# Scores of the next head pair ahead of VectorE's maxima, and w_out first in the queue, in a fused attention and two-MoE kernel

## What is computed

```python
q_d, k_d, v_d = (mean over groups of 4 positions of q, k, v)
out_up = np.repeat(sm_attn(q_d, k_d, v_d), 4, axis=2)      # pooled attention
mask = np.abs(pos[:, None] - pos[None, :]) < 4             # local attention
x = out_up + softmax(where(mask, q @ k.T / 8, -1e9)) @ v   # -> [2304, 512]
h = (sigmoid(x @ w_gate) * (x @ w_val)) @ w_out            # [2304, 512]
logits = h @ phi                                           # [2304, 32]
slots = softmax(logits, axis=0).T @ h                      # [32, 512]
slot_out[e] = relu(slots[e] @ w1[e]) @ w2[e]               # 8 experts, 4 slots each
out = softmax(logits, axis=1) @ slot_out
```

## Time and profile before

| | us |
|---|---|
| three runs, median (lowest to highest) | 636.86 (635.98 to 637.54) |
| the profiled execution, its own time | 634.59 |
| its span, first to last instruction | 632.8 |
| TensorE busy | 581.1 (92% of the span) |
| VectorE, ScalarE, GpSimd busy | 248.0, 221.7, 127.2 |
| mean granted TensorE clock | 0.948 of 2.4 GHz |

### The profile page before, as it was taken

The page is one execution under the profiler, slowest core; times in us unless marked ns, Lnnn a source line. Parts: engine busy times, 40 slices in busy tenths (PEclk is TensorE's granted clock), DMA queues, the critical chain, the costliest instruction groups (busy, mean ns, idle before and its releaser), DMA issues.

```text
span 632.8 us, 9888 instructions
## 1 busy us (share of the span) xinstructions
PE 581.1 (92%) x3719; PEld 458.3 (72%) x3719; DVE 248.0 (39%) x552; ACT 221.7 (35%) x559; POOL 127.2 (20%) x219
## 2 busy tenths in 40 slices
PE   4677989899999999999999999999999999958973
PEld 3466869688877888888888787888787787833431
DVE  2366246853545425253534443534311302130123
ACT  2555344545344332435242424333212222121113
POOL 8453230634122130313131121210000000000000
PEclk9899567999999999999999999999999999987997
DMA  9688331131131111111111020000530031999968
GB/s 210 200 233 232 53 78 44 34 77 48 30 77 38 41 38 40 38 40 39 40 38 39 21 58 20 22 0 21 185 149 1 1 134 63 398 351 402 394 254 298
DMA packets 86701, 70.87 MB, mean 112 GB/s; under 512 B 61312, under 2 KB 65920, under 8 KB 86656
## 3 DMA queue, kind: packets, MB, share of 16 engines
q1 hardware_dynamic: 86656, 70.25, 36.0%
HBM read 65.52 MB, written 4.72 MB: 111 GB/s over the span
## 4 chain that ended last, share of the span: by engine, by line
PE 82%; ACT 5%; DMA 4%; DVE 4%; issue 2%; SPq 2%; DVEq 0%; ACTq 0%
PE gateb L867 23%; PE valb L867 23%; PE unitb L824 5%; PE unitb L789 4%; PE unitb L875 4%; DMA ew_low<-in_moe_w_dram 3%; PE unitb L809 2%; PE unitb L896 2%; PE unitb L882 2%; PE unitb L816 2%; PE unitb L796 2%; PE unitb L942 2%; PE unitb L783 2%; PE gateb L960 1%; DMA xraw<-in_moe_w_out_dram 1%
## 5 line engine op out<-in xcount | busy, mean ns | idle before, releaser
L867 PE MATMUL gateb<-w_hl,xhl 128*128 128x512 f32 x648 | 162.7, 400 | 0.0
L867 PE MATMUL valb<-w_hl,xhl 128*128 128x512 f32 x648 | 161.6, 398 | 0.0
L867 PEld LDWEIGHTS gateb<-w_hl,xhl 128*128 128x128 f32 x648 | 119.2, 189 | 31.5 <-issue 7.7
L867 PEld LDWEIGHTS valb<-w_hl,xhl 128*128 128x128 f32 x648 | 117.8, 188 | 22.7
L600 ACT ACTIVATE hid<-gateb 128x512 f32<-128x512 f32 x54 | 32.3, 598 | 175.0 <-PE gateb L867 171.9
L717 DVE SCALAR_TENSOR_TENSOR hid<-hid,valb 128x512 f32<-128x512 f32 x54 | 37.1, 686 | 117.7 <-PE valb L867 117.6
L698 DVE TENSOR_TENSOR xraw<-unitb,outd 64x192 f32<-64x192 f32 x84 | 29.8, 355 | 51.3 <-PE unitb L824 50.3
L515 POOL TENSOR_TENSOR vd<-v 72x256 f32<-72x256 f32 x16 | 12.3, 770 | 168.3 <-PE unitb L809 157.7
L526 ACT ACTIVATE hT<-unitb 128x512 f32<-128x512 f32 (+1 forms) x66 | 36.6, 557 | 18.1 <-PE unitb L875 13.3
L510 POOL TENSOR_TENSOR qd<-qd,qblk 128x144 f32<-128x144 f32 x64 | 40.3, 629 | 5.0
L824 PE MATMUL unitb<-probT,vloc 70*128 70x128 f32 x252 | 34.8, 286 | 0.0
(11 more groups left out here) (193 smaller groups left out, 704.3 us busy)
## 6 DMA issues: line engine op xcount, KB each, us to landing
ew_low<-in_moe_w_dram SPq DMA_DIRECT2D x19, 1024.0 KB, 14.1
ew_high<-in_moe_w_dram SPq DMA_DIRECT2D x13, 1024.0 KB, 12.1
qtok<-in_q_dram SPq DMA_DIRECT2D x32, 144.0 KB, 2.9
ktok<-in_k_dram SPq DMA_DIRECT2D x32, 144.0 KB, 3.0
v<-in_v_dram SPq DMA_DIRECT2D x32, 144.0 KB
out_dram<-outs SPq DMA_DIRECT2D x18, 256.0 KB, 3.0
vloc<-in_v_dram SPq DMA_DIRECT2D x32, 112.0 KB
w_raw<-in_moe_w_gate_dram SPq DMA_DIRECT2D x6, 512.0 KB, 4.7
```

Of the source, the lines that this page charges most:

```text
L867: last = mm(bank[:, :], xhl[:, i % NX, x, kk, :], w_hl[:, c, m, w, kk, :], start=j == 0, stop=j == len(order) - 1)
```

## The change

Two things are changed. First, the order. VectorE's part of S0, S1 and Sd gets steps of its own (mx0, mx1, mxd), and so does ScalarE's part of Sd (exd) and exp (now ex). In the head S0 and S1 of the next pair now stand at the start of the turn, ahead of norm and the PT units of the present pair; mx0 and mx1 stand behind PT2; Q and K of the pair after the next stand behind Sd. The PV units are last but two. The body's order is the same but for three differences: S0 and S1 of pair 4 stand ahead of the first gate with their maxima behind it, three pieces are split at its start where there were two, and the list with more steps in it is spread anew. Second, SP's queue: w_out's first two pieces are loaded right after q and k of pair 0, two more before v's local rows, and the gate and value weights of chunks 1 and 2 after S1 of pairs 2 and 3 (before: 1 and 2).

```diff
-TURN = """norm S0+ S1+ PdT0 PdT1 Sd+ exp+ PT0 PVd PT1 pool_V+ norm_d+ Q++ PT2 PV0 PV1 K++ PV2"""
-HEAD_TURN = """S0 S1 WT PdT0- PdT1- exp PVd- pool_V Sd PV0- PV1- PV2- w_hi w_lo Q+ K+ GP WT norm norm_d GP
-               PT0 PT1 WT PT2 GP"""
+TURN = """norm S0+ mx0+ S1+ mx1+ PdT0 PdT1 Sd+ mxd+ exd+ ex+ PT0 PVd PT1 pool_V+ norm_d+ Q++ PT2 PV0 PV1 K++ PV2"""
+HEAD_TURN = """S0+ S1+ GP WT pool_V norm norm_d PT0 PT1 PT2 mx0+ mx1+ PdT0 PdT1 Sd+ Q++ K++ ex+ PVd mxd+ exd+ GP WT
+               w_hi w_lo PV0 PV1 PV2 GP WT"""
+LAST_TURN = """GP pool_V norm norm_d PT0 PT1 PT2 PdT0 PdT1 PVd PV0 PV1 PV2"""
...
-    split = [(name, n) for n in range(w_pieces // chunks, w_pieces) for name in ("w_hi", "w_lo")]
-    for n in range(len(split) // 4 - 1):
-        put(n, *split[4 * n + 4:4 * n + 8])
+    for n in range(sum(s[0] == "w_hi" for s in head), w_pieces):
+        step = [("w_hi", n), ("w_lo", n)]
+        if n < 6:
+            start += step
+        else:
+            put(n // 2 - 3, *step)
...
-            elif name == "Sd":
+            elif name == "exd":
+                ub, free = banks[at["Sd", arg][1]], bank_free[at["Sd", arg][1]]
                 act.wait_ge(maxd_done, arg + 1)
...
-            if name in ("S0", "S1"):
-                u = int(name[1])
+            if name in ("mx0", "mx1"):
+                u = int(name[2])
+                unit = (f"S{u}", arg)
+                ub, free = banks[at[unit][1]], bank_free[at[unit][1]]
                 t0, t1 = ((0, 5), (5, NQ))[u]
-                wait_unit(dve, s)
+                wait_unit(dve, unit)
...
             load_pair_qk(sp, 0, "q")
             load_pair_qk(sp, 0, "k")
-            load_v_pooled(sp, 0)
-            load_v_local(sp, 0)
+            for f in range(2):
+                load_wo_piece(sp, f)
             sp.dma_start(phi_sb[:, :, :], phi.rearrange("(k p) s -> p k s", p=P)).then_inc(phi_in, 16)
             for s in head:
                 sync_step(sp, s)
                 if s == ("K1", 0):
+                    load_v_pooled(sp, 0)
+                    for f in range(2, WO_STAGES):
+                        load_wo_piece(sp, f)
+                    load_v_local(sp, 0)
                     load_pieces(sp, 0)
-                    for f in range(WO_STAGES):
-                        load_wo_piece(sp, f)
-                if s[0] == "S1" and 0 < s[1] < FC:
+                if s in (("S1", 2), ("S1", 3)):
                     wait_unit(sp, s)
-                    load_pieces(sp, s[1])
+                    load_pieces(sp, s[1] - 1)
```

More of the change, by code:

```diff
@@ L32, with attention_steps @@
 EXTRA = ("w_hi", "w_lo", "WT", "GP")
-def attention_steps(pairs, turn, first):
+def attention_steps(turns, first, pairs):
     out, count = [], dict.fromkeys(EXTRA, 0)
-    for p in range(first - 2, pairs + 1):
+    for p, turn in turns:
         for token in turn.split():
-            name = token.rstrip("+-")
+            name = token.rstrip("+")
             if name in EXTRA:
-                if first <= p < pairs:
+                if p >= (0 if name[0] == "w" else -1) and not (name == "GP" and count["GP"] == count["WT"]):
                     out.append((name, count[name]))
@@ L45, in attention_steps @@
                 continue
-            own = p + token.count("+") - token.count("-")
+            own = p + token.count("+")
             if first <= own < pairs:
@@ L52, in program_steps @@
 def program_steps(tiles, chunks, batch_tokens, pairs, heads_of, w_pieces, wo_pieces):
-    head = attention_steps(heads_of + 1, HEAD_TURN, 0)
-    head = head[:head.index(("S0", heads_of))]
+    turns = [(p, HEAD_TURN) for p in range(-2, heads_of - 1)] + [(heads_of - 1, LAST_TURN)]
+    head = [s for s in attention_steps(turns, 0, heads_of + 1) if s[1] < heads_of or s[0] not in ("S0", "S1")]
     for n in range(wo_pieces // 4):
         head.insert(head.index(("GP", 4 * n + 3)) + 1, ("GS", n))
-    head += [(name, heads_of - 1) for name in ("PdT0", "PdT1", "PVd", "PV0", "PV1", "PV2")]
-    head += [("S0", heads_of), ("S1", heads_of)]
-    att = [s for s in attention_steps(pairs, TURN, heads_of) if s not in head]
+    done = set(head)
+    att = [s for s in attention_steps([(p, TURN) for p in range(heads_of - 2, pairs)], heads_of, pairs) if s not in done]
+    start = [("S0", heads_of), ("S1", heads_of), ("xs", 0)]
+    att = [s for s in att if s not in start]
     t0, t1 = tiles - 2, tiles - 1
@@ L107, in program_steps @@
         body += after[n]
-    return head[:-2] + [("xs", 0)] + head[-2:] + split[0:4], body
+    return head, start + body
 def place(head, body, narrow):
@@ L544, in act_step @@
                 copy(kT[:, t0 * TT:t1 * TT], ub[:, 0:(t1 - t0) * TT]).then_inc(free, 1)
-            elif name == "exp":
+            elif name == "ex":
                 act.wait_ge(sub_done, arg + 1)
@@ L648, in dve_step @@
                                         mask[:, t0:t1, :], ALU.add).then_inc(free, 1)
-                wait_free(dve, s)
+                wait_free(dve, unit)
                 nc.vector.reduce_max(mx[:, t0:t1], prob[:, arg % 2, t0:t1, :], AX.X).then_inc(max_done, 1)
@@ L655, in dve_step @@
                                             ALU.subtract).then_inc(sub_done, 1)
-            elif name == "Sd":
-                wait_unit(dve, s)
+            elif name == "mxd":
+                ub = banks[at["Sd", arg][1]]
+                wait_unit(dve, ("Sd", arg))
                 nc.vector.reduce_max(negd[:, :], ub[0:2 * DQ, 0:ND * SD].rearrange("p (t n) -> p t n", t=ND), AX.X,
```

## The result

The changed kernel takes **640.75 us** (median of 8 runs, 639.09 to 642.38), the kernel before 636.22 beside it (8 runs, 632.15 to 637.54): ratio 1.0084, 95% interval 1.0055 to 1.0113. It is slower by 0.8%, where a gain to 634.0 was forecast; 640.75 lies near the upper end of the stated 624 to 642. The profiled execution took 639.09, with a span of 637.3 and a mean granted clock of 0.934 (before: 634.59, 632.8, 0.948).

The account below looks back on a forecast made before the run. TensorE is busy nearly throughout 132.4 to 466 us, so only the first gate's time and the body's start could move: 634.59 − 3.9 + 1.0 = 631.7, or 634.0 on the median's scale; range 624 to 642.

Parts of the forecast that it names:

- S of pair 1 at: Head: with the w_out wait gone, the scores of pair 1 start at 21.8 us instead of 31.6.
- turn 1: Head, turn of pair 1: 2.8 us idle before GS, clock then lost, 23.25 us (17.46 before).
- turn 2: Head, turn of pair 2: GS stands later, waits for ScalarE's copies, 18.75 us (18.09 before).
- turn 3 to gate: Head, pair 3 until first gate: VectorE's norm holds last PT; 36.4 us at 1.2 GHz, 30.7 at 2.4, middle taken (34.1 before).
- body: Body's start: later maxima and splits give a 4 us wait before S0 of pair 5; net cost +1.0 us, rest unchanged.
- behind the body: Rest of the program after the last val unit: no change counted, 0 us.
- The one-turn case: Head: one turn alone fails to regain the clock, costing 2 to 5 us; 636 to 640 us, chance 0.15.
- rival (c): w_out wait goes, but new waits on banks, GS and late splits take it all; 636 to 638 us, chance 0.13.
- Rival (a): Clock never comes back in the head; gate at 110.1, time 646 us, chance 0.12.
- Rival (b): Clock stays at 2.4 GHz from the first turn on; gate at 82, time 620 us, chance 0.08.
- The chance of slower: Whole kernel: 0.31 that it measures slower than before, from rival (a), the one-turn case and some of rival (c).
- the 3.9 us of the head: Head: start and three turns sum to a first gate at 97.4 us, 3.9 ahead of 101.3.

Follow-up runs that it names:

- Exd early: Changed kernel with only mxd and exd moved right behind Sd, ahead of Q, in each turn: 637.97 us, ratio 1.0061.
- Filler: Changed kernel with unneeded transposes, 22 before the first GS and 20 before S0 of pair 5: 634.50 us; with 12 and 10 fp32 matmuls instead: 637.23 us.
- body as before: Changed kernel with the body's list in the order of the kernel before: 637.46 us, ratio 1.0029.
- queue only: Kernel before with the change's new loads of w_out and v alone, old order: 628.46 us (4 runs), then 629.54 (12 runs).
- GP early: Changed kernel with GP and GS ahead of Q and K in the turn, and mxd and exd ahead of ex and PVd: 635.05 us.
- queue only, filler: Kernel before with the new loads alone, plus 44 unneeded transposes in the 5.39 us wait before the second GP: 628.59 us.

## Why the prediction was wrong

Its sum for the profiled execution was 631.7 and the execution took 639.09. By its own terms:

| term | forecast | measured | error |
|---|---|---|---|
| S of pair 1 at | 21.8 | 20.5 | −1.3 |
| turn 1 | 23.25 | 22.8 | −0.5 |
| **turn 2** | 18.75 | 22.6 | **+3.8** |
| turn 3 to gate | 33.55 (36.4 and 30.7 halved) | 35.8 | +2.3 |
| **body** | +1.0 | +5.0 | **+4.0** |
| behind the body | 0 | −0.9 | −0.9 |

**Turn of pair 2** is the step that failed. I took it as "same start to 12.45, WT 12.9, PV 14.9", without asking which unit had PV0's bank before. I had followed banks for PdT1 and Sd only. Where no GS stands between Sd and PV0, as in turn 2, the ring of eight gives PV0 the bank of Sd, whose reader, exd, now stands late in ScalarE's row. The wait is 2.18 us, and the clock falls with it (0.55 from 58.26 to 61.90), which makes PV 3.90 us. *Exd early* shows it: with mxd and exd moved and nothing else, the turn is 18.9. *Filler* shows that most of the 3.8 us is the clock: with the wait but without the loss of clock it is 19.2.

**Turn 1** was right in mechanism and size: the forecast had 2.8 us idle before GS on ScalarE's copy and the clock lost, the trace has 3.13 and 0.50. So were the end of the w_out wait and a wait on VectorE's `prob` before Sd, of 0.47 us; the one before PdT1, forecast at 0.55, doesn't show in this turn.

**Turn 3**: I took the middle of two clock cases, a time that neither gives. The measured 35.8 is near the slow one, 36.4, but that is in part luck: the clock was not at 0.50 throughout, as it was at 0.99 from 72.2 to 82.6, and TensorE stood idle for 2.23 us before PV0, which I didn't have. That idle stretch is gone in *exd early*, where the last PT instead waits 1.85 us for VectorE's norm, as I had it, and the turn takes 36.1. So the bank is not what makes turn 3 long.

**The body's start** was followed to the right place (S0 of pair 5 at 14.9 us behind the gate; measured 116.92 − 101.70 = 15.2) and priced too low. I counted the wait and set against it the idle time that it would take in later. The clock was left out: behind the wait val(0,1) takes 4.69 us for 3.00. Idle time is only 1.6 longer. The first gate's 1.3 us (5.17 for 3.90) is clock too, but not a cost of the body's order: it takes 4.8 to 5.2 us in *body as before* and in four of the five profiles of the old order with the new queue. With it at the lower clock the old body lasts 455.4 to 455.9, so the new body's order costs some 3.6 to 4.1 of the 5.0. Of the idle time some stands at one later place, an LG unit whose bank waits for exd, which I had taken as zero:

```profile
175.94 1.50 PE L893 MATMUL unitb<-hT,gmat 128*32 128x256 f32 x24 [1.22 <-ACT probd L560]
```

In the kernel before this unit had no wait. The filler at S0 of pair 5 took away val's part (body 456.4 with a gate unit of 3.88 us, at a clock of 0.75, and 457.6 with one of 5.06), the old body order all but the gate unit's (455.9).

**The rivals.** The one-turn case (636 to 640, 0.15) is the nearest to what came, one turn failing by 3.8 us, though by a bank and not by luck of the clock. By its mechanism rival (c) is nearer (636 to 638, 0.13): the w_out wait went, and the new waits took all of it in the head. It had nothing more for the body's start, and was 3 us low. Rival (a) did not hold: the clock came back at about 28 us (0.53 from 26 to 28, then 1.00), at about 52, behind WT, PT and PdT units (0.51 from 43.3 to 52, then 1.00), and once more at about 72 (0.50 from 65.9 to 72.2, then 0.99). Rival (b) didn't either. The chance of slower, 0.31, was too low for a reason that the rows had: they showed the clock lost behind a stretch with a wait of 2 us, and the new order added waits at three places.

**The queue half** would have been a good forecast alone. I had only the sum: with the 3.9 us of the head I took order and queue as one gain, while the order cost 6.1 us there, against the first profile of queue only (gates at 101.7 and 95.6), and 11.4 against the second (90.3). It gave the queue's gain back.

What stays open: why turn 3 took 34.1 to 34.4 us, at a mean clock of 0.55, in three kernels of the old order and in the kernel before, and 27.0 and 28.9, at 0.82 and 0.73, in two profiles of queue only, one of them behind a turn 1 at 0.89. One profile of each kernel can't tell a rule from a draw.

## What to carry to other kernels

When a reader of a buffer is moved to a later place, follow every unit that gets that buffer next, in every turn in which the ring falls differently; a wait of 2 us on one bank went with a turn 3.7 us longer where the clock fell with it, and only 0.3 longer in the one profile in which the clock held. Price a new wait on TensorE twice, as idle time and as the clock behind it: 3.1 us before GS cost 3.7 more in the work that followed. Try the parts of a change alone: here a queue edit worth −7 us was hidden by an order edit worth +12. The kernel to keep is the old order with the new queue (629.54, 12 runs), with the split moved behind norm_d (626.19, 6 runs).

## What the runs showed of the hardware

- Transposes kept the clock up as well as matmuls did. 22 of them in 2.62 us, ahead of a wait of 0.58, left GS and PV at a granted clock of 1.00, as 12 fp32 matmuls in 2.94 us did ahead of a wait of 0.26; without filler it was 0.50. 44 of them in the 5.39 us wait left the clock at 1.00, where both profiles without them had 0.50 behind it. This was measured for fp32 of 128x128 between other units, and for holding the clock; whether transposes alone would raise it was not tried.
- Executions of one program differ more than its steps do. *GP early* ran from 629.82 us at a mean granted clock of 0.958 to 639.18 at 0.931, and the last part of the program took 76.1 us at a clock of 0.90 in the changed kernel and 79.4 at 0.84 in *queue only, filler*, for identical instructions. A profile is one draw of the clock; an effect of 3 us is read from medians, or from a stretch in which both kernels run at the same clock.
